# The first batch's attention cut at 232 queries for 348, its token chunks at 232 and 344, and the opening laid out anew

## What is computed

```python
q_d, k_d, v_d = (a.reshape(B, H, S // 4, 4, D).mean(axis=3) for a in (q, k, v))
out_up = np.repeat(softmax(scale * q_d @ k_d.T) @ v_d, 4, axis=2)      # pooled, 144 groups
scores = np.where(abs(i - j) < 4, scale * q @ k.T, -1e9)
out_local = softmax(scores) @ v                                        # a band of 7 keys
x = (out_up + out_local) as (2304, 512)
h = maximum(maximum(x @ w1, x @ w2), x @ w3); y = h @ w_out            # 512 -> 768 -> 512
g = y @ w_in2; out = maximum(0.01 * g, g) @ w_out2                     # 512 -> 2048 -> 512
```

## Time and profile before

| | us |
|---|---|
| median of 3 runs | 772.4 (771.91 to 772.46) |
| the profiled execution | 771.94, its span 770.2 |
| TensorE busy | 762.8 (99%) |
| VectorE, ScalarE, GpSimd busy | 446.5, 296.3, 167.0 |
| DMA mean | 128 GB/s |
| granted clock of TensorE | 1.00 |

### The profile page before, as it was taken

The page is one execution under the profiler, slowest core; times in us unless marked ns, Lnnn a source line. Parts: engine busy times, 40 slices in busy tenths (PEclk is TensorE's granted clock), DMA queues, the critical chain, the costliest instruction groups (busy, mean ns, idle before and its releaser), DMA issues.

```text
span 770.2 us, 13539 instructions
## 1 busy us (share of the span) xinstructions
PE 762.8 (99%) x5412; PEld 684.7 (89%) x5412; DVE 446.5 (58%) x769; ACT 296.3 (38%) x697; POOL 167.0 (22%) x208
## 2 busy tenths in 40 slices
PE   9999999999999999999999999999999999999998
PEld 7889989888888889999998988989898998889896
DVE  6867797666745463765756566564434466334433
ACT  4675544333242323433544354442222244222222
POOL 3795121211111333340435533110000000000000
PEclk9999999999999999999999999999999999999999
DMA  8642432332121023212567644446432236223402
GB/s 286 212 161 96 138 119 80 103 96 71 49 76 37 1 68 120 66 44 85 169 254 262 257 178 151 191 152 215 158 118 96 96 133 236 96 97 107 156 25 83
DMA packets 37630, 98.91 MB, mean 128 GB/s; under 512 B 2880, under 2 KB 23360, under 8 KB 34496
## 3 DMA queue, kind: packets, MB, share of 16 engines
q1 hardware_dynamic: 37568, 98.05, 36.4%
HBM read 73.92 MB, written 24.12 MB: 127 GB/s over the span
## 4 chain that ended last, share of the span: by engine, by line
PE 95%; DVE 2%; ACT 1%; issue 1%; DMA 1%; SPq 0%; DVEq 0%; ACTq 0%
PE mlp_ps L1067 10%; PE mlp_ps L1069 9%; PE mlp_ps L1068 9%; PE mlp_ps L1219 8%; PE mlp_ps L1221 8%; PE mlp_ps L1220 8%; PE att_ps L1240 6%; PE att_ps L1242 6%; PE att_ps L1241 6%; PE mlp_ps L1242 3%; PE mlp_ps L1241 3%; PE mlp_ps L1240 3%; PE att_ps L1139 2%; PE att_ps L1141 2%; PE att_ps L1140 2%; PE att_ps L1056 2%
## 5 line engine op out<-in xcount | busy, mean ns | idle before, releaser
L1067 PE MATMUL mlp_ps<-x_hi,wa_lo 128*128 128x288 f32 (+1 forms) x288 | 101.7, 353 | 0.1
L1069 PE MATMUL mlp_ps<-x_hi,wa_hi 128*128 128x288 f32 (+1 forms) x288 | 97.4, 338 | 0.0
L1068 PE MATMUL mlp_ps<-x_lo,wa_hi 128*128 128x288 f32 (+1 forms) x288 | 97.1, 337 | 0.0
L1507 ACT ACTIVATE h_last_a<-wa_raw 128x384 fp32r<-128x384 f32 x72 | 37.8, 524 | 104.7 <-DVE wa_raw L1841 104.1
L1067 PEld LDWEIGHTS mlp_ps<-x_hi,wa_lo 128*128 128x128 f32 x288 | 54.0, 188 | 6.0 <-DVE x_raw L1676 0.3
L1839 DVE TENSOR_TENSOR wa_raw<-mlp_ps,h_raw 128x384 f32<-128x384 f32 x24 | 13.4, 557 | 79.1 <-PE mlp_ps L1221 51.4
L1069 PEld LDWEIGHTS mlp_ps<-x_hi,wa_hi 128*128 128x128 f32 x288 | 54.1, 188 | 4.6
L1068 PEld LDWEIGHTS mlp_ps<-x_lo,wa_hi 128*128 128x128 f32 x288 | 54.3, 188 | 4.0
L1853 DVE TENSOR_TENSOR h_last_b<-wa_raw,h_last_a 128x384 fp32r<-128x384 f32 x72 | 43.3, 605 | 23.5 <-ACT h_last_a L1507 21.1
L855 POOL TENSOR_TENSOR v_rows<-v_rows 72x512 f32<-72x512 f32 x16 | 21.0, 1312 | 152.2 <-DMA v_rows<-in_v_sum 152.2
L1242 PE MATMUL att_ps<-wa_hi,h_last_a 128*128 128x512 f32 x132 | 52.2, 396 | 0.0
(11 more groups left out here) (215 smaller groups left out, 2049.1 us busy)
## 6 DMA issues: line engine op xcount, KB each, us to landing
u_even<-u_scratch SPq DMA_DIRECT2D x8, 1792.0 KB, 7.4
u_odd<-u_scratch SPq DMA_DIRECT2D x8, 1792.0 KB, 7.3
kq_in<-in_kq SPq DMA_DIRECT2D x14, 576.0 KB, 3.9
u_scratch<-u_even SPq DMA_DIRECT2D x4, 1792.0 KB, 8.7
u_scratch<-u_odd SPq DMA_DIRECT2D x4, 1792.0 KB, 9.7
v_rows<-in_v_sum SPq DMA_DIRECT2D x16, 288.0 KB
wa_raw<-in_w SPq DMA_DIRECT2D x6, 768.0 KB, 6.3
v_win<-in_v_band SPq DMA_DIRECT2D x12, 384.0 KB, 3.6
```

The costliest lines, as they stand in the source:

```text
L1067: nc.tensor.matmul(ps, wlo, xhi, start=(n == 0), stop=False)
L1068: nc.tensor.matmul(ps, whi, xlo, start=False, stop=False)
L1069: last = nc.tensor.matmul(ps, whi, xhi, start=False, stop=(n == len(pairs) - 1))
L1507: nc.scalar.activation(g_tile(0, quad, part), g_raw[part], ACT.Copy).then_inc(g_hi_ready, 1)
```

## The change

Front units take blocks 0 and 1 (232 queries, 58 groups), back units blocks 2, 3 and 4 (86 groups). v's windows are laid out for this. Chunks 0 and 1 have 232 and 344 tokens. The first load of k and q is two DMAs, of the first 240 columns (`KQ_FIRST`) and the rest, with the sums of unit 0 in two parts, and `pooled_scores` waits for one more count. Only unit 0 does its local scores ahead of the pooled ones (before, units 0 and 1). Unit 2's transposes use `FRONT_BANK`. `N` is split: `NG` is ScalarE's part, with a place of its own. The opening's order is new (zeros, loads, G and W halves among it), and the positions of the later units are shifted.

```diff
 WHOLE, FRONT, BACK = "whole", "front", "back"
-PART_SLOTS = {WHOLE: ((0, 1, 2, 3, 4), (1, 0, 3, 2, 4)), FRONT: ((0, 1, 2), (1, 0, 2)), BACK: ((3, 4), (3, 4))}
-PART_MASK = {WHOLE: (0, 5), FRONT: (0, 3), BACK: (3, 5)}
-PART_GROUPS = {WHOLE: ((0, 72), (72, 72)), FRONT: ((0, 87),), BACK: ((87, 57),)}
+PART_SLOTS = {WHOLE: ((0, 1, 2, 3, 4), (1, 0, 3, 2, 4)), FRONT: ((0, 1), (0, 1)), BACK: ((2, 3, 4), (3, 2, 4))}
+PART_MASK = {WHOLE: (0, 5), FRONT: (0, 2), BACK: (2, 5)}
+PART_GROUPS = {WHOLE: ((0, 72), (72, 72)), FRONT: ((0, 58),), BACK: ((58, 86),)}
 UNITS = ([(p, FRONT) for p in range(PAIRS)] + [(p, BACK) for p in range(PAIRS)]
          + [(p, WHOLE) for p in range(PAIRS, NPAIR)])
 NU = len(UNITS)
+KQ_FIRST = -(-(Q_START[2 * PART_MASK[FRONT][1] - 1] + TQ) // FACTOR) * FACTOR
 BACK0, WHOLE0 = PAIRS, 2 * PAIRS
...
-PART_OUT = {WHOLE: (((0, 2), 4), ((1, 3), 4)), FRONT: (((0,), 2), ((1,), 2)), BACK: (((3,), None), ((4,), None))}
-V_BLOCKS = {WHOLE: ((0, 1, 4, 5, 8, 9), (2, 3, 6, 7, 8, 9)), FRONT: ((0, 1, 4, 5, 6, 7), (2, 3, 4, 5, 8, 9))}
+PART_OUT = {WHOLE: (((0, 2), 4), ((1, 3), 4)), FRONT: (((0,), None), ((1,), None)), BACK: (((2,), 4), ((3,), 4))}
+V_BLOCKS = ((0, 1, 4, 5, 8, 9), (2, 3, 6, 7, 8, 9))
 NV = 6
-PART_V = {WHOLE: (0, 6), FRONT: (0, 4), BACK: (4, 6)}
+PART_V = {WHOLE: (0, 6), FRONT: (0, 2), BACK: (2, 6)}
 def out_column(part, r, bp):
...
 def v_index(part, r, t):
     lo, hi = PART_V[part]
-    return lo + V_BLOCKS[WHOLE if part == WHOLE else FRONT][r][lo:hi].index(t)
+    return lo + V_BLOCKS[r][lo:hi].index(t)
...
-CHUNK = [(0, 288), (288, 288)] + [(S + 480 * i, 480) for i in range(2)]
+CHUNK = [(0, 2 * BLOCKS2), (2 * BLOCKS2, S - 2 * BLOCKS2)] + [(S + 480 * i, 480) for i in range(2)]
 WIDE = 480
 NC1 = len(CHUNK)
 GROUPS = [("h", f, w) for f in range(NF1) for w in range(3)] + [("y", f, 0) for f in range(KM)]
...
-    put(0, ("LQ", 0), ("LQ", 1), ("LR", 0), ("LQ", 2), ("LV", 0), ("LR", 1), ("LQ", 3), ("LV", 1), ("WL", 0),
-        ("Z", 8), ("D", 0), ("D", 1), ("S", 0), ("Z", 5), ("E", 0), ("D", 2), ("G", 0), ("S", 1), ("Z", 6), ("E", 1),
-        ("LR", 2), ("G", 1), ("N", 0), ("S", 2), ("Z", 2), ("T", 0), ("Z", 3), ("E", 2), ("D", 3), ("LR", 3), ("WL", 1),
-        ("V", 0), ("W", 0, 0), ("W", 0, 1), ("LV", 2), ("XH", 0, 0), ("N", 1), ("XL", 0, 0), ("S", 3), ("Z", 2), ("G", 2), ("T", 1),
-        ("Z", 3), ("E", 3), ("G", 3), ("W", 1, 0), ("N", 2), ("V", 1), ("Z", 8), ("LV", 3), ("WL", 2), ("T", 2), ("XH", 0, 1), ("N", 3),
-        ("W", 1, 1), ("XL", 0, 1), ("Mk", 0, 0, 1), ("Mk", 1, 0, 1), ("Mk", 2, 0, 1), ("V", 2), ("T", 3), ("D", 4),
-        ("Mk", 0, 1, 2), ("Mk", 1, 1, 2), ("Mk", 2, 1, 2), ("LV", 4), ("WL", 3), ("X", 0, 2),
-        ("V", 3), ("D", 5), ("LV", 5), ("WL", 4), ("WL", 5), ("Mk", 0, 2, 3), ("Mk", 1, 2, 3), ("Mk", 2, 2, 3),
-        ("X", 0, 3), ("S", 4), ("E", 4), ("Mk", 3, 0, 3))
+    put(0, ("LQ", 0), ("LQ", 1), ("LR", 0), ("LQ", 2), ("LV", 0), ("WL", 0), ("LR", 1), ("LQ", 3), ("LV", 1),
+        ("Z", 8), ("D", 0), ("S", 0), ("Z", 8), ("E", 0), ("D", 1), ("G", 0), ("N", 0), ("NG", 0), ("S", 1), ("E", 1), ("D", 2),
+        ("Z", 1), ("T", 0), ("W", 0, 0), ("G", 1), ("LR", 2), ("WL", 1), ("N", 1), ("Z", 6), ("V", 0), ("LV", 2), ("WL", 2),
+        ("NG", 1), ("XH", 0, 0), ("D", 3), ("S", 2), ("XL", 0, 0), ("LR", 3), ("WL", 3), ("Z", 1), ("T", 1), ("E", 2), ("N", 2),
+        ("Z", 4), ("V", 1), ("LV", 3), ("NG", 2), ("W", 0, 1), ("XH", 0, 1), ("S", 3), ("G", 2), ("T", 2), ("E", 3), ("XL", 0, 1),
+        ("N", 3), ("W", 1, 0), ("G", 3), ("Z", 6), ("V", 2), ("LV", 4), ("WL", 4), ("NG", 3), ("XH", 0, 2),
+        ("Mk", 0, 0, 1), ("Mk", 1, 0, 1), ("Mk", 2, 0, 1), ("T", 3), ("XL", 0, 2), ("W", 1, 1),
+        ("Mk", 0, 1, 2), ("Mk", 1, 1, 2), ("Mk", 2, 1, 2), ("V", 3), ("LV", 5), ("WL", 5), ("D", 4), ("XH", 0, 3),
+        ("Mk", 0, 2, 3), ("Mk", 1, 2, 3), ("Mk", 2, 2, 3), ("XL", 0, 3), ("S", 4), ("E", 4), ("D", 5), ("Mk", 3, 0, 3))
     for i in range(NF1):
         put(4, ("WL", NF1 + i))
-    for c, at in ((2, 0.5), (3, 2.4), (4, 5.4), (5, 8.4)):
+    for c, at in ((2, 0.2), (3, 2.4), (4, 4.8), (5, 7.5)):
         put(at, ("W", c, 0))
         put(at + 1, ("W", c, 1))
-    for c, at in ((6, 10.3), (7, 11.3), (8, 12.7), (9, 13.7), (10, 14.7), (11, 15.7)):
+    for c, at in ((6, 10.3), (7, 11.3), (8, 12.3), (9, 13.3), (10, 14.3), (11, 15.3)):
         put(at, ("W", c, 0))
     put(0, ("LQ", 4))
-    put(2.2, ("S", 5), ("E", 5))
+    put(2.3, ("S", 5), ("E", 5))
     put(1.5, ("LQ", 5))
-    plan = {4: (3.1, 6.0, 7.0, 8.6), 5: (7.6, 9.6, 10.4, 12.0), 6: (11.0, 12.8, 13.8, 15.6), 7: (14.4, 16.4, 20.1, 18.3),
-            8: (18.5, 21.2, 22.4, 24.2), 9: (22.6, 25.2, 26.2, 28.2), 10: (26.2, 29.5, 30.5, 32.5), 11: (31.2, 34.5, 35.5, 37.5),
+    plan = {4: (2.2, 5.4, 6.6, 8.0), 5: (7.3, 9.4, 10.6, 12.0), 6: (11.3, 13.4, 17.8, 15.6), 7: (14.6, 17.0, 21.3, 18.9),
+            8: (20.6, 22.8, 24, 25.8), 9: (24.3, 26.6, 27.6, 29.4), 10: (27.9, 30.6, 31.6, 33.4), 11: (32, 34.7, 35.7, 37.5),
             12: (36.5, 40, 41.6, 43.7), 13: (43, 45.8, 46.7, 48.4), 14: (47.6, 50.3, 51.2, 52.9), 15: (52.1, 54.8, 55.7, 57.4),
             16: (57.5, 59.3, 62, 63.8), 17: (62.6, 65.6, 66.5, 68.3), 18: (67.4, 70.1, None, 72.4), 19: (71.9, 74.6, None, 76.4)}
     for u, (n_at, t_at, s_at, v_at) in plan.items():
...
         if part == WHOLE:
             put(n_at - 2, ("LR", p))
             put(n_at, ("G", p))
-        put(n_at, ("N", u))
+        put(n_at, ("N", u), ("NG", u))
         put(t_at, ("T", u))
         if s_at is not None:
             put(s_at - (1.95 if u == PAIRS + 3 else 1.5), ("D", u + 2))
...
 def stage_jobs(item):
     kinds = STAGE_JOBS.get(item[0], ())
-    return kinds[2:] + kinds[:2] if item[:2] in (("S", 0), ("S", 1)) else kinds
+    return kinds[2:] + kinds[:2] if item[:2] == ("S", 0) else kinds
 def bank_of(kind, u):
-    if u < 2 or (kind, u) == ("lt0", PAIRS - 1):
+    if u < 2 or u == 2 and kind in STAGE_JOBS["T"] or (kind, u) == ("lt0", PAIRS - 1):
         return FRONT_BANK.get(kind, JOB_BANK[kind])
     return JOB_BANK[kind]
...
         _last[BANKS + group_bank(NG1)] = ("c11", SQ - 1)
 JOBS = len(JOB)
-LT = {WHOLE: ((0, 3), (3, 5)), FRONT: ((0, 3),), BACK: ((0, 2),)}
+LT = {WHOLE: ((0, 3), (3, 5)), FRONT: ((0, 2),), BACK: ((0, 3),)}
 def combines(part):
...
         att_ps = ctx.enter_context(nc.psum_tensor("att_ps", [P, 4, 512], F32))
         mlp_ps = [ctx.enter_context(nc.psum_tensor(f"mlp_ps{i}", [P, 512], F32)) for i in range(BANKS)]
+        kq_first_loaded = sem("kq_first_loaded")
         kq_loaded = [sem(f"kq_loaded{i}") for i in range(PAIRS)]
         v_loaded = [sem(f"v_loaded{i}") for i in range(2)]
         vwin_loaded = [sem(f"vwin_loaded{i}") for i in range(2)]
...
                 if p >= PAIRS:
                     sp.wait_ge(att_done, JOB["sl1", p if p < PAIRS + 2 else p + 2] + 1)
-                sp.dma_start(kq_of(p), kq[divmod(p, PAIRS)]).then_inc(kq_loaded[p % PAIRS], 16)
+                src = kq[divmod(p, PAIRS)]
+                if p == 0:
+                    sp.dma_start(kq_of(0)[:, :, 0:KQ_FIRST], src[:, :, 0:KQ_FIRST]).then_inc(kq_first_loaded, 16)
+                    sp.dma_start(kq_of(0)[:, :, KQ_FIRST:S], src[:, :, KQ_FIRST:S]).then_inc(kq_loaded[0], 16)
+                else:
+                    sp.dma_start(kq_of(p), src).then_inc(kq_loaded[p % PAIRS], 16)
             def load_v_rows(p):
                 if p >= 2:
...
             def local_scores(u):
                 p, part = UNITS[u]
                 lo, hi = PART_MASK[part]
-                pe.wait_ge(kq_loaded[p % PAIRS], 16 * (p // PAIRS + 1))
+                if u == 0:
+                    pe.wait_ge(kq_first_loaded, 16)
+                else:
+                    pe.wait_ge(kq_loaded[p % PAIRS], 16 * (p // PAIRS + 1))
                 begin(("sl0", u))
                 begin(("sl1", u))
                 ps = [bank("sl0", u), bank("sl1", u)]
...
                         pe.wait_ge(mask_ready, 3)
                     for h in range(2):
                         nc.tensor.matmul(ps[h][:, 0:(hi - lo) * TQ], ident[:, :],
-                                         mask[:, SLOTS // 2 * h + lo:SLOTS // 2 * h + hi, :].rearrange("p s w -> p (s w)"),
+                                         mask[:, lo:hi, :].rearrange("p s w -> p (s w)"),
                                          start=False, stop=True).then_inc(att_done, 1)
             def pooled_scores(u):
                 p, part = UNITS[u]
-                pe.wait_ge(sums_ready, u + 1)
+                pe.wait_ge(sums_ready, u + 2)
                 begin(("sg0", u))
                 begin(("sg1", u))
                 gs = [bank("sg0", u), bank("sg1", u)]
...
                             last.then_inc(att_done, 1)
             def scores(u):
-                if u < 2:
+                if u == 0:
                     local_scores(u)
                     pooled_scores(u)
                 else:
...
             for item in FIRST:
```

(15 more changed lines are left out.)

## The result

The changed kernel takes **791.1 us** (median of 4 runs, 789.29 to 791.77) beside 772.43: a ratio of 1.0236, 95% interval 1.0216 to 1.0256. It is slower by 19 us, where 3 were forecast. The profiled execution is 791.29, its span 789.5.

The account below looks back on a forecast made before the run. It took TensorE's own queue to bound the kernel after the opening. Masks -1.0, opening +3.0, wait at 41 -0.9, new waits +1.6 and widths +0.5 gave +3.2 on 771.94: 775.1 us, eight in ten from 769.5 to 779.5.

Parts of the forecast that it names:

- The opening, +3.0: Up to the end of `Mk` 3: zeros and waits on TensorE grow from 15.7 to 18.7 us, +3.0.
- One more DMA issue ... so it costs nothing: SP's queue: the split load's extra issue delays no later load, since these wait for transfers ahead; 0, or 0.4 us uncovered.
- the walk: Step-by-step timing of the opening's engine queues from the profile's durations, error about 0.7 us; it gave the +3.0.
- GpSimd's order: Opening: sums of v alternate with weight halves on GpSimd, so values 1 and 2 wait; the main reason for +3.0.
- The faster rival: Opening: GpSimd does not hold the values, G2 ends ahead of 22.3 and TensorE never waits; about 769.6 us, chance 0.25.
- The clock: Rival, opening: TensorE's clock falls to 1.2 GHz in the pause, pieces up to values 3 double; +1.7, 776.9 us, chance 0.12.
- The wait at 41, -0.9 and +1.6: Chunk 0: an earlier `NG` 4 removes the wait at unit 4's transposes, -0.9; new waits there add +1.6, between 0 and 2.5.
- Widths, +0.5: Chunks 0 and 1: products take 110 ns at 232 columns and 158 at 344, +0.5 us; bounds 0 and +7.2.
- little to spare just where the change makes TensorE's work shorter: From 34.7 to 50.9 us: ScalarE, GpSimd and VectorE are nearly full; ScalarE is busy 13.1 of 16.2 us.
- Later units, 0: From chunk 1 on: due times from unit 8 move by some tenths of a group or earlier; cost 0.
- The split's own gain: Opening: with the first load in two parts, unit 0's local scores start earlier, worth 0.2 us.
- masks: Front units: mask products shrink from 192 to 128 columns, -1.0 us of TensorE work over four units.

Follow-up runs that it names:

- e7: The changed kernel with the first load of k and q as one DMA again: 786.99 us, ratio 1.0174.
- e2: The changed kernel with 42 more zero matmuls in four places of the opening: 789.94 us, ratio 1.0226.
- e3: The changed kernel with GpSimd's sums of v 1, 2 and 3 each ahead of the weight half beside it: 786.06 us, ratio 1.018.
- e5: The kernel before with only its first two chunks cut at 232 and 344 tokens for 288 and 288: 776.13 us, ratio 1.0051.

## Why the prediction was wrong, point by point

- **The opening, +3.0: mechanism right, size wrong.** It measured +11.4. The step that failed first is "One more DMA issue ... so it costs nothing": the cut alone costs 3.9 us on before and 4.8 in the changed kernel. Pair 1's sums start at 9.07, where the walk had 7.9 and e7 8.22, and the load of pair 3, which the walk took as landed, was 2.76 late. Every later number of the walk inherits this, W 0 0 at 16.35 for 13.6, values 1 at 20.65 for 18.3, values 2 at 29.38 for 25.1, values 3 at 35.88 for 29.7. With the single load (e7) they are 13.94, 18.39, 24.99 and 30.07. Of the 8.4 us that the opening is longer than forecast, 6.2 are there at values 3. The other 2.2 lie between there and the end of `Mk` 3, at 41.66 for 33.3, and are mostly half clock: e2, at full clock, is 1.6 shorter there.
- **GpSimd's order.** The step named the right queue and the right waits, and e3 prices the order at 4.3 us with an error of 2, against 3.0 in the sum. The faster rival asked where G2 ends, before 22.3 or not; it ended at 29.3.
- **The clock.** It fell to the 1.2 GHz level at about 20 us, as that rival said, after TensorE had been busy 2.55 of 5 us, and stayed there to about 40. Products then start 0.213 apart for 0.112. Its price of 1.7 was the right size: e2's opening is 2.1 shorter, and its time 0.8, with an error of 2. But the rival let the pieces up to values 3 double, and those were mostly hidden; the cost came behind them, where it had the clock back.
- **The wait at 41, -0.9 and +1.6.** Unit 4's probabilities were there in time, as said, and the waits from 42 to 60 us were 1.30 for low parts, 0.51 for copies and 0.36 for the sum of a unit. That is 2.2, near the 1.6. Unit 4's transposes did not wait for `E` 5. But the forecast looked no further than scores 7, and 3.75 us of waits and about 1.6 of half clock stand between 75 and 92 us.
- **Widths, +0.5.** The spacing was right: 112 ns at 232 columns (25 steps from 44.07 to 46.87) for 110, and 158 to 159 at 344 (22 steps from 100.99 to 104.48) for 158, so 1.1 us. The step that failed is that the width was priced as products alone. The Trainium skill ("TensorE: Matmul & The Clock Gate", Back-to-back issue gap) would have given 99 ns at 232 as the bare gap; no run here comes under 110. The other 2.8 us of e5 are waits for ScalarE and VectorE. That they come from as much work beside a chunk that is a fifth shorter is my reading; no run lightens that work. The prediction named the same reason ("little to spare just where the change makes TensorE's work shorter") and counted it only for 38 to 52 us.
- **Later units, 0: wrong.** "Due times from unit 8 on move by some tenths of a group" passed over the number in unit 6's row. A row's third number is the scores of the unit two later: 13.8 became 17.8, four groups. It cost 4.6 us: the waits of 1.13 and 1.76, and the half clock behind them. Rows 8 to 10 did not move by tenths either, but by 0.9 to 2.1 groups later (18.5 to 20.6 at the most), and unit 8's transposes then wait 1.33 at 96.30.
- **No earlier start.** The split's own gain was put at 0.2, and it brought nothing: unit 0's scores start at 4.90 before, after and in e7.

By ratios: split 4.8 (3.9 on before), unit 8's scores 4.6, GpSimd's order 4.3, widths 3.9, weights' load 0. That is 17.6 of 18.2 (0.0236 of 772.3), each with an error of 1.2 to 2.5, so that masks, zeros, unit 8's row and the rest lie within it, and that the sum comes so close is in part luck. What stays open: how the split load costs, through its small packets or through the longer and later issues, as both came together in every run with it; and whether any plan makes 232 and 344 as fast as 288 and 288. None of those tried did.

## What to carry to other kernels

Cutting the first of a queue of loads moved every load behind it here; ask where the last of them lands and who waits, not when the first piece comes. In a list that orders several in-order engines, a due time is an order: before moving an item, list what it passes on each engine, and above all do not let work that is ready fall behind an instruction that waits (here exps behind a division). A stage made shorter for one engine keeps the other engines' work, so price the whole stage at its fullest engine. A wait can cost more than its length where TensorE sets the pace, since its clock may fall behind it (here 3 to 7 us at half clock behind waits of 1 to 2 us). And read every number of a changed table, since the one that was passed over cost as much as the term that the walk was spent on.

## What the runs showed of the hardware

- A load of 576 KB cut in 240 and 336 KB slowed the issue of the next load too (0.43 to 0.60 us) and the rate of the first ten us by 15 to 22% (188 and 354 GB/s to 146 and 301), and pair 1's sums started 2.1 us later. The Trainium skill ("DMA: Bandwidth & Descriptors", Bandwidth, Measured) advises DMAs of 1 MiB and more, from a table of loads that GpSimd issues, where these are SyncE's; by that alone both forms are small, and no run here separates size from the rest.
- TensorE stayed at the 1.2 GHz level from about 20 to 40 us although it was busy 10.00 of 10 us from 30 on (granted clock 0.50 in that window).
- What half the clock costs depends on who sets the pace. In the opening some twenty us of it, most beside waits, cost 2.1 us at the end of `Mk` 3 (41.66 for e2's 39.52). In chunk 0, where TensorE sets the pace, products of 232 columns start 0.213 us apart for 0.112 for 3 us in the changed kernel, about 7 in e2 and e3 and about 6 in e7. By these two spacings that costs nearly half of the time in which it works, an estimate.
